# First half of w_in ahead of v, smaller first chunks of q and k, column sums before the last two chunks, and a new place for v's first tile

## What is computed

```
qn = q / (norm(q, over rows) + 1e-6);  kn = k / (norm(k, over rows) + 1e-6)     # q, k, v: 6016 x 256
s  = kn.T @ qn / tau;  A = softmax(s, last axis)                              # 256 x 256
x  = v @ A
h  = x @ w_in;   g = s * relu(h)**2 + b;                  x = g @ w_out        # w_in 256 x 2048
h2 = x @ w_in2;  g = max(h2, 0) + alpha * min(h2, 0);     out = g @ w_out2     # w_out 2048 x 256
```

## Time and profile before

| | |
|---|---|
| median of 3 runs | 1036.84 us (1035.64 to 1036.85) |
| profiled execution, its own time | 1036.88 us |
| span of that execution | 1035.1 us |
| PE busy | 1027.3 us (99%) |
| DVE busy | 848.2 us (82%) |
| ACT busy | 617.0 us (60%) |
| POOL busy | 52.3 us (5%) |
| start of the first layer product | 56.82 us |

### The profile page before, as it was taken

One profiled execution on the slowest core, in us unless ns is written; L12 is line 12 of the kernel. 1 busy time (PEld: TensorE's weight loads), 2 busy tenths in 40 slices (PEclk: granted clock), 3 DMA queues, 4 the chain that ended last, 5 costly groups with the idle time before them and its releaser, 6 DMA issues.

```text
span 1035.1 us, 13263 instructions
## 1 busy us (share of the span) xinstructions
PE 1027.3 (99%) x4583; PEld 858.2 (83%) x4583; DVE 848.2 (82%) x1281; ACT 617.0 (60%) x1029; POOL 52.3 (5%) x78
## 2 busy tenths in 40 slices
PE   9999999999999999999999999999999999999997
PEld 7868888888888888888998888888888888888997
DVE  6888888889788888788998888777768777877875
ACT  5577776666566566566676665455545455445553
POOL 1021000000000000000661000000000000000000
PEclk9999999999999999999999999999999999999999
DMA  9853303302402211300741606004103203200201
GB/s 360 260 81 61 62 1 122 62 1 82 102 1 82 82 19 41 120 1 31 251 136 54 244 1 181 3 1 154 30 1 143 41 1 125 41 1 0 42 0 37
DMA packets 129891, 79.12 MB, mean 76 GB/s; under 512 B 98128, under 2 KB 106528, under 8 KB 129824
## 3 DMA queue, kind: packets, MB, share of 16 engines
q1 hardware_dynamic: 124960, 71.63, 23.1%
q0 software_dynamic: 3712, 6.30, 2.8%
q10 hardware_dynamic: 1152, 0.34, 0.1%
HBM read 50.54 MB, written 27.72 MB: 76 GB/s over the span
## 4 chain that ended last, share of the span: by engine, by line
PE 97%; ACT 1%; DVE 1%; DMA 1%; issue 0%; SPq 0%; ACTq 0%
PE acc L467 16%; PE acc L469 16%; PE acc L468 16%; PE hab L467 8%; PE hab L469 8%; PE hab L468 8%; PE hcd L467 6%; PE hcd L469 6%; PE hcd L468 6%; PE acc L570 3%; PE acc L592 1%; DMA qk_raw<-in_k_dram 1%; SPq L326 0%; PE hcd L592 0%; PE hab L592 0%
## 5 line engine op out<-in xcount | busy, mean ns | idle before, releaser
L754 ACT ACTIVATE g_hi<-cb 128x512 fp32r<-128x512 f32 (+1 forms) x384 | 233.7, 620 | 194.8 <-DVE cb L986 123.5
L469 PE MATMUL acc<-g_hi,wo_lo 128*128 128x512 f32 (+1 forms) x766 | 295.2, 385 | 0.0
L467 PE MATMUL acc<-g_hi,wo_hi 128*128 128x512 f32 (+1 forms) x766 | 295.2, 385 | 0.0
L468 PE MATMUL acc<-g_lo,wo_hi 128*128 128x512 f32 (+1 forms) x766 | 295.1, 385 | 0.0
L992 DVE TENSOR_TENSOR g_lo<-cb,g_hi 128x512 fp32r<-128x512 f32 (+1 forms) x384 | 247.2, 685 | 41.3 <-ACT g_hi L754 39.3
L469 PEld LDWEIGHTS acc<-g_hi,wo_lo 128*128 128x128 f32 x766 | 143.8, 188 | 27.1
L468 PEld LDWEIGHTS acc<-g_lo,wo_hi 128*128 128x128 f32 x766 | 143.8, 188 | 27.1
L467 PEld LDWEIGHTS acc<-g_hi,wo_hi 128*128 128x128 f32 x766 | 143.8, 188 | 26.8
L986 DVE SCALAR_TENSOR_TENSOR cb<-cb,alph 128x512 f32<-128x512 f32 (+1 forms) x192 | 142.2, 741 | 20.9 <-ACT cb L724 14.8
L467 PE MATMUL hab<-x_hi,ws_hi 128*128 128x512 f32 (+1 forms) x384 | 149.7, 390 | 0.0
L468 PE MATMUL hab<-x_lo,ws_hi 128*128 128x512 f32 (+1 forms) x384 | 148.0, 385 | 0.0
(11 more groups left out here) (129 smaller groups left out, 962.6 us busy)
## 6 DMA issues: line engine op xcount, KB each, us to landing
x_dram<-x_hi SPq DMA_DIRECT2D x35, 256.0 KB, 2.4
x_dram<-x_lo SPq DMA_DIRECT2D x35, 256.0 KB, 2.7
x_hi<-x_dram SPq DMA_DIRECT2D x35, 256.0 KB, 5.1
x_lo<-x_dram SPq DMA_DIRECT2D x35, 256.0 KB, 5.3
qk_raw<-in_q_dram SPq DMA_DIRECT2D x10, 512.0 KB, 11.1
qk_raw<-in_k_dram SPq DMA_DIRECT2D x10, 512.0 KB, 12.7
out_dram<-y_sq SPq DMA_DIRECT2D x40, 128.0 KB, 2.8
v_raw<-in_v_dram SPq DMA_DIRECT2D x36, 128.0 KB, 3.3
```

Source lines behind the costliest of these rows:

```text
L467: pe.matmul(dst, w_hi, m_hi, start=start, stop=False, skip_group_check=True)
L468: pe.matmul(dst, w_hi, m_lo, start=False, stop=False, skip_group_check=True)
L469: return pe.matmul(dst, w_lo, m_hi, start=False, stop=stop, skip_group_check=True)
L754: sc.activation(g_hi[:, blk, 0:w], cb[:, blk, 0:w], ACT.Copy).then_inc(g_hi_done[blk], 1)
```

## The change

1. **Chunks.** `ROWS_OF` goes from 2, 2, ten times 4, 2, 1 to 1, 2, 2, 3, nine times 4, 2, 1: 15 chunks where there were 14. `FOLD_AT` moves from chunk 8 to the last but one, so whole chunks of four rows are added in one instruction, and the fold to two rows stands behind the last of them.
2. **Column sums of q and k.** PE forms them before the scores of the last two chunks (2 rows and 1 row), where they stood between these two.
3. **Scalars and alpha.** Their small products go to a bank of `hcd`. DVE copies the scalars behind the reciprocals, and alpha and its signs between the first and the second logits; both were done in the middle of the squares.
4. **v's first tile** is turned behind the reciprocals, where it was turned before them. The x_low of its first part moves from before the first logits to behind them.
5. **ACT** makes the first two x_high behind `rq_row`, no more ahead of the exponential's table.
6. **w_in.** SP loads its first half ahead of v.
7. **w1.** The first of the two products of block 1 goes ahead of the second turn of A.
8. **Column sums of w_out.** PE's products in step 7 and two waits are gone. POOL folds `wsum` over the partitions with seven accumulating transfers, each waiting for the one before, stores the row in memory, waits, and loads it as a column with two transfers. DVE reads that.

```diff
-ROWS_OF = (2, 2) + (CHUNK,) * 10 + (2, 1)
+ROWS_OF = (1, 2, 2, 3) + (CHUNK,) * 9 + (2, 1)
...
-FOLD_AT, PART = 8, CHUNK // 2
+FOLD_AT, PART = CHUNKS - 2, CHUNK // 2
...
-        scal_ps = acc[1][:, 0, 16:20]
-        alpha_ps = acc[1][:, 0, 32:32 + NF]
+        scal_ps = h_d[:, 16:20]
+        alpha_ps = h_d[:, 32:32 + NF]
...
             for i in range(CHUNKS):
                 load_chunk(i)
+            load_win(0)
             load_v(0, 0)
             load_v(0, 1)
-            for g in range(2):
-                for b in range(CB):
-                    sp.dma_start(win[:, g:F // WQ:2, b, :],
...
+            load_win(1)
...
+            pool.wait_ge(wsum_whole, 1)
+            for i in range(7):
+                half = P >> i + 1
+                wait(pool, wsum_folded, 16 * i)
+                pool.dma_start(wsum[0:half, 0, :], wsum[half:2 * half, 0, :], accum_op=ALU.add).then_inc(wsum_folded, 16)
+            pool.wait_ge(wsum_folded, 16 * 7)
+            pool.dma_start(colsum_dram.rearrange("(a c) -> a c", a=1), wsum[0:1, 0, :]).then_inc(colsum_stored, 16)
+            pool.wait_ge(colsum_stored, 16)
+            for b in range(CB):
+                pool.dma_start(colsum[:, b:b + 1], colsum_dram[b * P:(b + 1) * P].rearrange("(p a) -> p a", a=1)).then_inc(colsum_ready, 16)
...
-                if n == STEPS - 1:
-                    pe.wait_ge(c21_read, STEPS - 1)
-                    pe.wait_ge(wsum_whole, 1)
-                    for b in range(CB):
-                        mm = pe.matmul(colsum_ps[:, b:b + 1], wsum[:, 0, b * P:(b + 1) * P], ones[:, 0:1],
-                                       start=True, stop=True)
-                    mm.then_inc(colsum_ready, 1)
...
             w1_block(0)
+            w1_block(1, (0,))
             turn_a(1)
-            for i in range(1, W1_EARLY):
+            w1_block(1, (1,))
+            for i in range(2, W1_EARLY):
                 w1_block(i)
...
             sc.activation(root, cols_ps[:, 0:4], ACT.Sqrt, bias=tiny).then_inc(root_ready, 1)
-            x_high(0, 0)
-            x_high(0, 1)
             sc.activation(unused[:, 1:2], ones[:, 0:1], ACT.Exp)
             sc.wait_ge(rq_ready, 1)
             sc.activation(rq_row[:], rq_ps, ACT.Copy).then_inc(rq_copied, 1)
+            x_high(0, 0)
+            x_high(0, 1)
...
                 if n == STEPS - 1:
-                    ve.wait_ge(colsum_ready, 1)
-                    ve.tensor_scalar(bias2, colsum_ps, scal[:, 2:3], None, ALU.mult).then_inc(bias2_ready, 1)
+                    ve.wait_ge(colsum_ready, 16 * CB)
+                    ve.tensor_scalar(bias2, colsum[:], scal[:, 2:3], None, ALU.mult).then_inc(bias2_ready, 1)
```

48 lines of the change are left out of this document (26 added, 22 removed).

## The result

| | before | changed |
|---|---|---|
| median | 1036.24 us (1035.64 to 1037.57, 22 executions) | 1038.07 us (1036.96 to 1041.27, 22 executions) |
| profiled execution, its own time | 1036.88 us | 1037.81 us |
| span of it | 1035.1 us | 1036.0 us |
| start of the first layer product | 56.82 us | 57.58 us |

The ratio is 1.0017 [1.0011, 1.0023]: the changed kernel is slower by 1.8 us, less than the 0.2% that was set as the bound of "no change", but its interval doesn't reach 1. Its highest executions lie much further from its lowest than those of before: nine of the 22 took over 1038.2 us, a time that no execution of before reached.

The account below looks back on a forecast made before the run. PE was taken to bound the kernel, with 97% of the chain of waits. +0.82 - 0.47 = +0.35 us on 1036.88 gave 1037.2 us; own range 1036.4 to 1038.1, over all cases 1035.2 to 1038.9.

Parts of the forecast that it names:

- The squares: Ahead of q and k's column sums: squares whole at 42.25 us, 0.45 later than before, so PE waits 1.3 us.
- The lead: Scores of q and k: smaller first chunks put PE two products, 0.87 us, ahead, lost in the wait for the squares.
- The rival of late first loads: Eight issues for the first 2 MB, not six, make the data late: 1037.7 to 1038.7 us; chance 0.12.
- rq_diag, logits, second turn: Head: rq_diag's product about 46.1 us, logits 47.14 and 51.69, second turn of A 53.47; +0.82 us for all that follows.
- DVE's slack ahead of the first step: Ahead of step 0: DVE is 1.68 us late, slack taken to cover 0.86 us; without it the term is +1.68.
- w_in ahead of v: Load order: w_in sooner is worth nothing, v comes 2.6 us later but DVE's new order covers it; cost 0.
- The late v of the rivals: v's first tile comes over 1.1 us later than estimated; at 2 to 3 us more, 1038 to 1039; chance 0.02.
- The column sums of w_out: Around 133 us: four records leave PE, -0.47 us; POOL's nine steps at 4.4 us each are in time, cost 0.
- the rival in which POOL comes late: At DVE's bias: steps over 5.1 us make DVE wait; at 5.6 us, 4 us late, 1041 us; chance 0.06.
- The step that failed: At q and k's column sums: start 0.44 us sooner, line 623 two products (0.87 us) later in order, net +0.43 us.
- The sum's base: The whole span: the sum starts from 1036.88 us, the profiled execution of before, close to the 1036.84 median of three runs.

Follow-up runs that it names:

- a2_foldearly: The changed kernel with the fold of the squares back ahead of chunk 4, pieces of two rows from there: 1036.26 us, ratio 1.0001.
- b1_colsum: The kernel before with item 8 alone (column sums of w_out by POOL's transfers): 1035.96 us, ratio 0.9999.
- f1_colhalf: The kernel before with items 8 and 7 alone (w_out's column sums on POOL, half of w1's block 1 sooner): 1035.23 us, ratio 0.9992.
- f3_best: The kernel before with items 8, 7 and the chunks of item 1, fold at chunk 4, scalars and alpha behind chunk 2: 1034.61 us, ratio 0.9988.
- d1_colsback: The changed kernel with the column sums of q and k back between the last two chunks (item 2 undone): 1036.78 us, ratio 1.0007.
- e1_combo: The changed kernel with the fold ahead of chunk 4, and alpha and signs behind the second logits: 1035.85 us, ratio 1.0001.
- a1_winlate: The changed kernel with both halves of w_in behind v again (item 6 undone): 1037.29 us, ratio 1.0017.
- r_after: The changed kernel once more, no edit, for a second profile: 1037.26 us, ratio 1.0015.
- a3_alphearly: The changed kernel with alpha and signs copied in the middle of the squares again, behind chunk 6: 1037.58 us, ratio 1.0014.
- c1_filler: The changed kernel with two products whose result nobody reads, ahead of PE's wait for the squares: 1037.07 us, ratio 1.0015.
- f2_both: The changed kernel with the fold ahead of chunk 4, and alpha and signs behind chunk 2: 1035.13 us, ratio 0.9993.
- g1_idle: The kernel before with two clearings by DVE ahead of its last fold, so that PE idles: 1041.02 us (5 executions), ratio 1.0045.

## Why the prediction was partly right

The forecast was 1037.2 us and "no change"; the median is 1038.07, inside the range, and the ratio within 0.2%, though on the slower side. That it lies inside is partly luck: the base was 0.64 us too high and the loss 1.48 us too small. By its own steps:

- **The squares** were to be whole at 42.25 us and PE to start its sums at 42.3. They were whole at 42.00 and 42.20 us in the two traces, and the sums started at 42.06 and 42.26. Right, and for the reason given: the start of the last full chunk is set by the data (ACT 33.66, waiting 0.65), so the moved fold stands bare at the end. a2_foldearly, which moves it back alone, has them at 40.92. Wrong was what this was set against. The forecast lets the sums start 0.44 us sooner than before, at 42.3 for 42.74; but 42.74 is the end of the scores in one late execution. Against b1_colsum and f1_colhalf (41.95 and 41.93 us) the sums of the changed kernel start 0.1 to 0.3 us *later*.
- **The lead** of 0.87 us differs between executions: in the second trace PE had done the scores at 40.67 us (16.23 + 24.44; 41.00 forecast) and idled 1.59 us (1.3 forecast), in the first, where row 7's data came 0.7 us later than in before, there is next to none. It is worth nothing while the squares set the start; with a2_foldearly's fold and before's order it is gained (f3_best, scores ended at 41.24 us for the 42.12 of b1_colsum).
- **The rival of late first loads** came to little: with the new chunks PE went on late in two traces (10.68 and, in d1_colsback, 10.81 us), but in both traces of the changed kernel ACT began the last full chunk at 33.66 and 33.86 us, no later than the 33.92 of before. Its remark that no row shows loads of 128 KB in this queue is wrong: the earlier trace rows has four of them (`v_first`).
- **rq_diag, logits, second turn**: forecast 46.1, 47.14, 51.69 and 53.47 us; measured 46.08, 47.14, 51.64 and 53.41. The first product was to come 0.82 us later and came 0.76 later. The reading of DVE's row between the logits was right, three alph and sign steps included. Part of the closeness is luck, though: the forecast sets 42.3 against the end of the scores, where the row of the sums starts at 42.58, and the squares came 0.25 us sooner than it said; the two errors nearly cancel. And against b1_colsum's first product (56.18 us) it is 1.40 us late.
- **DVE's slack ahead of the first step** was taken to cover what DVE is late. It did in the changed kernel (0.76 us late at the first product and 0.77 at 70 us); e1_combo shows where it ends, 0.74 us of wait at `ws_lo`.
- **w_in ahead of v**, forecast at 0: right (a1_winlate). The late v of the rivals did not come: DVE turned its first tile at 45.57 us without a wait.
- **The column sums of w_out**, forecast -0.47 us on PE: right (+0.76 falls to +0.3 behind 134 us; b1_colsum has -0.45 there). The forecast and the rival in which POOL comes late had the price of a step wrong: it is 1.8 to 3.7 us, not 4.4. The nearest row by kind was a poor guide; that transfer moves 256 KB from memory, these 64 KB and less. The Trainium skill, "DMA: Bandwidth & Descriptors", section "Anatomy of one DMA", gives 2.0 us plus the bytes, and its estimate of about 110 us was the closer one to the 114 us here.
- **The step that failed** is "-0.44 + 0.87 = +0.43 us. The lead of 0.87 us is lost in that wait." It prices PE's wait at its own length. The wait also brings the granted clock down in some executions (r_after: 0.50 for more than three microseconds, 1.7 us more on 14 records), so the first trace was forecast within 0.1 us up to the first product, but not the spread above it. The second fault of the step is its base, the late profile of before: with b1_colsum's head in its place the loss is not +0.82 but +1.40 us. In r_after the four executions above 1038.2 us have a granted clock of 0.996 or 0.997 over the whole, the seven below it 0.999 or 1.0. The effect on the clock is also seen in how the kernels divide: over 1038.2 us were 9 of 22 and 4 of 11 of the changed kernel, 5 of 11 of a3_alphearly and of a1_winlate, which keep the late fold; one of 11 of c1_filler; none of a2_foldearly, b1_colsum, d1_colsback, e1_combo, f1_colhalf, f2_both and f3_best, and none of before. A fixed bound favours the kernels that are faster, but these are also narrower: 1.1 to 2.0 us from lowest to highest (f2_both 2.75, for one execution at a clock of 0.999), where the changed kernel has 4.2 and 4.3. f2_both and e1_combo have an idle time of 0.81 and 0.48 us at that place in their traces and none over the bound, while a1_winlate has 1.31 us in a trace at full clock. So neither any gap nor each long one does it; how long the gap was in the executions without a trace is not known.
- **The sum's base** was 1036.88 us, the profiled execution of before; its median turned out 1036.24. That alone makes the forecast 0.64 us too high, and the late head of that execution is as much. The loss beside the median is +1.83 us, where +0.35 was forecast.

**How the 1.83 us divide.** Shown: +0.76 in the head and -0.45 at 133 us in an execution at full clock, both against the profile of before, and some 1.7 to 2.1 us more in the one traced execution of this kernel in which the clock fell. The median over the 22 is 1038.07, over the 13 that are not above 1038.2 it is 1037.55; so by this estimate the clock adds about 0.5 us to the median. That leaves 1037.55 - 1036.24 = 1.3 us for undisturbed executions. The terms that the traces show come near it once the head is set against b1_colsum's: 57.58 - 56.18 = 1.40 us in the head, less the 0.45 at 133 us, is 0.95. That b1_colsum's head is the usual one of before is likely, not shown: three of four traces have it, and g1_idle's undisturbed execution lies above before's median by what its delay against b1_colsum is (2.76 and 2.72 us). Another 0.3 us stand in both traces of the changed kernel between 972 and 992 us: +0.47 grows to +0.79 in the first, 2.34 to 2.68 in the second. They come of a slower pace of the products there (see the last section), with no wait in it and no edit near. Whether the change has to do with that pace was not settled. Nor was why the undisturbed executions of r_after are nearer to before (the seven lower ones have a median of 1036.66 us, 0.6 over it) than those of the first measurement.

## What to carry to other kernels

- Before a work item is moved behind the last of a series, ask what arrives last. An engine that waits for data can't use saved time ahead of it, and all that is moved behind the last arrival stands bare: the fold cost nothing in the middle and 1.1 us at the end.
- A gap in PE's stream is to be priced with what it may do to the granted clock behind it, from executions beside the profiled one. Where a median moves more than its trace, look at the clock of every execution and profile the kernel a second time.
- Of two waits in a row the later one decides what the earlier is worth, and work moved past a wait is often owed at the next: e1_combo moved three small steps to behind the second logits and paid 0.8 us for a gain of 0.5 at `ws_lo`.
- A single profile is one execution. Here the base profile was 0.6 us late in its head, more than the change's whole forecast. Before differences of tenths are added up, compare the base with a second trace of the same instructions.

## What the runs showed of the hardware

- **The clock after short gaps.** Behind an idle time of 1.59 us (r_after) the granted clock went from 1.00 to 0.50, which is 1.2 GHz, about 2.3 us after PE had resumed, although PE was busy meanwhile, and came back near 48 us. In between stood the column sums, eight small products of one column. With 2.53 us (g1_idle) it fell before PE had resumed at 44.67 us (0.65 on average from 44 to 45 us) and stayed down until past 51 us. Behind 1.31 us (a1_winlate), and behind 0.32 us in the first trace of the changed kernel, it stayed up. The Trainium skill, "TensorE: Matmul & The Clock Gate", section "What's actually happening", says that the number of products at the slow clock differs from run to run in one kernel, there at a kernel's start; a gap in the middle is another case, but there too two executions of one kernel differ here: none of the 14 records behind it was slow in the first trace (3.27 us, after 0.32 us idle), and 1.7 us were lost on them in r_after (4.95 us, after 1.59).
- **Small accumulating transfers** within the chip's own buffer, issued by POOL, took 1.8 us (1 KB) to 2.1 us (32 KB) to landing in the changed kernel, the 256 KB ones from memory 4.4 us. The same transfer differs by a microsecond between executions: the one of 64 KB took 3.4 us there and 3.6 in r_after, but 2.3 in b1_colsum and 2.4 in f3_best, and the one of 4 KB took 3.0 us there, but 1.9 in r_after and f3_best.
- **Two paces of the same products.** The products of 448 columns follow each other at one of two distances, at a granted clock of 1.00 in both. From 978 to 988 us before and a2_foldearly start 51 of them in 10.14 us, 0.203 us each; the changed kernel, r_after and c1_filler 50 in 10.13, 10.12 and 10.13 us, 0.207 each. From 1004 to 1014 us before has the slower pace too (50 from 1003.81 to 1013.94), and a2_foldearly still the faster one (51 from 1003.72 to 1013.86). Against a2_foldearly it cost before 0.6 us of its span by the end and the changed kernel 0.9 to 1.0. No edit reaches that part. In the traces of a1_winlate, a3_alphearly, b1_colsum, d1_colsback, e1_combo, f2_both, f3_best and g1_idle the faster pace holds to the end; f1_colhalf goes over to the slower one near 1004 us. The cause stayed open, and one trace per kernel cannot tell a kernel's pace from an execution's; so spans of single profiles were not used for differences under a microsecond, only the places in the head.
